# The set-up of a three-stage kernel, reordered: three K buffers, value sums on TensorE, the expert-embedding norm moved into attention, one activation table set, other queue orders

## The reference

```python
# stage A: attention over a window of |i-j| < 16 and 24 block summaries per head
k_sum = k.reshape(B, H, nb, 32, D).max(axis=3)      # 24 blocks of 32 rows
v_sum = v.reshape(B, H, nb, 32, D).mean(axis=3)
scores = concat(masked(q @ k.T / sqrt(D)), q @ k_sum.T / sqrt(D) + log(32))
x = softmax(scores) @ concat(v, v_sum)              # (1536, 512)
# stage B: top-1 of 8 experts
xn, en = x / (norm(x) + 1e-6), expert_emb / (norm(expert_emb) + 1e-6)
expert = argmax(xn @ en.T / tau);  gate = max softmax probability
x = gate * (relu(x @ w1[expert]) @ w2[expert])      # 512 -> 1024 -> 512
# stage C: a rational activation
h = x @ w_in                                        # 512 -> 2048
out = (P(h) / (Q(|h|) + 1e-6)) @ w_out              # -> (1536, 512)
```

## Time and profile before

| | us |
|---|---|
| three runs | 852.5, 858.95, 860.91 |
| median of them | 858.95 |
| profiled execution, whole time | 860.77 |
| its span, first to last instruction | 859.2 |
| PE busy | 711.8 |
| DVE busy | 514.1 |
| ACT busy | 432.4 |
| POOL busy | 162.0 |

### The profile page before, as it was taken

How to read it: one execution, slowest core, us unless ns; L and a number is a source line. 1 busy time by engine, 2 the same in 40 slices (tenths; PEclk the granted TensorE clock), 3 DMA queues, 4 the chain that set the end, 5 groups by cost and what they waited for, 6 DMA issues and landing times.

```text
span 859.2 us, 12541 instructions
## 1 busy us (share of the span) xinstructions
PE 711.8 (83%) x3368; PEld 563.4 (66%) x3369; DVE 514.1 (60%) x922; ACT 432.4 (50%) x783; POOL 162.0 (19%) x210
## 2 busy tenths in 40 slices
PE   0586995999308888889899988479999999999995
PEld 0564774777206666768678767357778677878884
DVE  4861662566503646631331330479999899989996
ACT  3461662466304556532432442466666666666663
POOL 5756662431150000010101000310100000000000
PEclk9785997899658998999989999779999999999999
DMA  6134352440344668730541250210000100010001
GB/s 221 56 114 154 111 143 53 107 104 15 125 180 173 229 229 289 266 127 33 205 161 49 77 187 17 67 56 13 26 13 0 49 0 0 0 50 0 1 2 49
DMA packets 54380, 80.54 MB, mean 94 GB/s; under 512 B 31168, under 2 KB 31168, under 8 KB 53064
## 3 DMA queue, kind: packets, MB, share of 16 engines
q1 hardware_dynamic: 45144, 54.39, 19.7%
q0 software_dynamic: 6112, 20.45, 6.9%
q10 hardware_dynamic: 3088, 5.26, 1.7%
HBM read 63.48 MB, written 16.61 MB: 93 GB/s over the span
## 4 chain that ended last, share of the span: by engine, by line
PE 48%; DVE 19%; DMA 11%; ACT 9%; issue 5%; SPq 3%; POOL 3%; ACTq 1%; DVEq 0%; POOLq 0%
PE bank L1290 13%; PE bank L1117 8%; DMA xg<-x_by_slot 8%; PE bank L1269 6%; PE bank L1343 5%; PE bank L1358 5%; PE bank L1205 3%; SPq L340 3%; PE bank L1179 3%; DVE qd L1073 3%; DVE pb L1075 3%; DVE rr L1074 3%; ACT rr L755 2%; PE bank L1204 2%; DVE qd L1066 2%
## 5 line engine op out<-in xcount | busy, mean ns | idle before, releaser
L1358 PE MATMUL bank<-weights,G 128*128 128x512 f32 x576 | 144.4, 400 | 5.9 <-DVE G L998 5.8
L1343 PE MATMUL bank<-X2T,weights 128*128 (+1 forms) x576 | 145.8, 403 | 1.6 <-DVE X2T L998 1.6
L1358 PEld LDWEIGHTS bank<-weights,G 128*128 128x128 f32 x576 | 108.9, 190 | 34.1 <-DVE G L998 5.7
L1343 PEld LDWEIGHTS bank<-X2T,weights 128*128 128x128 f32 x576 | 109.8, 192 | 28.6 <-issue 2.3
L1290 PE MATMUL bank<-weights,HT 128*128 x456 | 122.2, 428 | 2.4 <-DVE HT L998 2.4
L1269 PE MATMUL bank<-weights,XT 128*128 (+1 forms) x456 | 116.4, 405 | 5.7 <-DVE XT L998 5.7
L1290 PEld LDWEIGHTS bank<-weights,HT 128*128 128x128 f32 x456 | 92.8, 207 | 24.4 <-issue 2.6
L1269 PEld LDWEIGHTS bank<-weights,XT 128*128 128x128 f32 x456 | 85.2, 191 | 27.4 <-issue 8.8
L998 DVE TENSOR_TENSOR HT<-bank,HT 128x512 fp32r<-128x512 f32 x38 | 24.5, 686 | 101.3 <-ACT HT L700 101.2
L755 ACT ACTIVATE rr<-qd,onep 128x512 f32<-128x512 f32 x48 | 34.9, 727 | 51.9 <-DVE qd L1066 51.9
L998 DVE TENSOR_TENSOR weights<-raw_early,weights 128x2048 f32 (+1 forms) x18 | 40.5, 2289 | 32.7 <-ACT weights L679 21.8
(11 more groups left out here) (180 smaller groups left out, 1246.0 us busy)
## 6 DMA issues: line engine op xcount, KB each, us to landing
raw_early<-in_moe_w_dram SPq DMA_DIRECT2D x14, 1024.0 KB, 5.1
raw_late<-in_moe_w_dram SPq DMA_DIRECT2D x14, 1024.0 KB, 8.8
x_by_slot<-x_all ACTq DMA_DIRECT2D x5, 1024.0 KB, 5.1
xg<-x_by_slot POOLq DMA_DIRECT2D x19, 256.0 KB, 5.6
y_by_slot<-yo POOLq DMA_DIRECT2D x19, 256.0 KB, 2.3
x_all<-in_moe_w_dram POOLq DMA_DIRECT2D x8, 512.0 KB, 5.3
kraw<-in_k_dram SPq DMA_DIRECT2D x3, 1024.0 KB, 5.3
qraw<-in_q_dram SPq DMA_DIRECT2D x12, 256.0 KB, 4.6
```

Of the source, the lines that this page charges most:

```text
L1343: last = T_.matmul(bank[6 + f % 2][:, :], W[:, 0, wa, kc * F2 + f * P:kc * F2 + (f + 1) * P], X2T[:, bass.ds(c % 2, 1), xa, kc * C_TOK:(kc ...
L1358: last = T_.matmul(bank[tt][:, :], G[:, f % 2, ga, tt * P:(tt + 1) * P], W[:, 1, wa, f * DM:(f + 1) * DM], start=(f == 0 and n_ == 0), sto ...
```

## The change

Eight edits, all ahead of stage B but one.

1. `kraw` gets three buffers. `load_k(2)` moves up behind `load_q(0)` and waits for nothing. ACT's `key_halves(2)` moves ahead of `key_columns(1)`; DVE's `key_max` is cut in two parts, and `key_max(2)` and `key_maxima(2)` move into the attention loop (DVE units 0 and 1, PE and ACT unit 4).
2. The value sums of groups 0 and 1 move from POOL to PE: four matmuls of 512 columns by the identity into one bank (`value_sums`), and a reduction and a scaling on DVE (`mean_v` on DVE). Group 2 stays on POOL, later.
3. The embedding norm moves into attention: ACT unit 0, DVE units 2 and 3, PE unit 3.
4. `Sqrt` becomes `Ln` and `Exp` with scale 0.5, and one table set is loaded at the start; the load ahead of stage C goes.
5. `DVE_FILLS` goes from two fills of a group to one.
6. POOL: `windows(0)` ahead of `split_q(1)`, `split_q(2)` and `windows(2)` ahead of the constants; the splits of expert 0's weights are spread over tiles 3 to 8, two in tiles 4 and 6.
7. SP: `load_q(T + 1)` ahead of `load_v(T)`.
8. SP: the `VA` load of the first tile of a batch is cut in two, 80 rows and 9.

The scratch row of `square_sum` becomes `x_all[T + 1]`, so `make_x(T)` waits for `ss_done` of T.

```diff
@@ sync
-                if g >= 2:
-                    sp.wait_ge(kmax_ready, g - 1)
-                sp.dma_start(kraw[:, g % 2, :], k_rows[g * P:(g + 1) * P, :]).then_inc(k_in[g], 16)
+                sp.dma_start(kraw[:, g, :], k_rows[g * P:(g + 1) * P, :]).then_inc(k_in[g], 16)
...
+                split = mid if cut == 0 else FIRST_ROWS
+                at = NSUM + split - start
+                sp.dma_start(heads(VA[NSUM + cut:at, r, :]),
+                             v[b, :, start + cut:split, :].rearrange("h p d -> p h d")).then_inc(v_in[r], 16)
+                if split < mid:
+                    sp.dma_start(heads(VA[at:P, r, :]),
+                                 v[b, :, split:mid, :].rearrange("h p d -> p h d")).then_inc(v_in[r], 16)
...
             load_q(0)
+            load_k(2)
             load_v_all(0)
             load_v_all(1)
             load_q(1)
-            load_k(2)
             sp.wait_ge(cleared, 1)
             load_v(0)
             load_v(1)
             store_means(0)
-            load_v_all(2)
             store_means(1)
             load_means(0)
             load_means(1)
+            load_v_all(2)
+            load_q(2)
             store_means(2)
             for T in range(2, NT):
-                load_q(T)
+                if T + 1 < NT:
+                    load_q(T + 1)
                 load_v(T)
@@ gpsimd
             split_q(0)
-            mean_v(0)
-            mean_v(1)
-            split_q(1)
             windows(0, 0)
             windows(0, 1)
+            split_q(1)
             windows(1, 0)
             windows(1, 1)
+            split_q(2)
+            windows(2, 0)
             mean_v(2)
+            windows(2, 1)
             load_raw(0)
             load_raw(1)
...
-            split_slab0(0)
-            for T in range(2, NT):
+            SPLITS = {3: (0,), 4: (1, 2), 5: (3,), 6: (4, 5), 7: (6,), 8: (7,)}
+            for T in range(3, NT):
                 split_q(T)
                 windows(T, 0)
                 windows(T, 1)
-                if T < 2 * CHUNKS + 1:
-                    split_slab0(T - 1)
+                for j in SPLITS.get(T, ()):
+                    split_slab0(j)
@@ scalar
+            A_.preload_act_table_set("natural_log_exp_and_others")
+            def norm_of_embedding():
...
+                A_.activation(sm[0:E, 1:2], sm[0:E, 0:1], ACT.Ln).then_inc(emb_log, 1)
+                act.wait_ge(emb_log, 1)
+                A_.activation(sm[0:E, 1:2], sm[0:E, 1:2], ACT.Exp, scale=0.5).then_inc(emb_root, 1)
...
+            key_halves(2)
             key_columns(1)
             key_maxima(1)
-            key_halves(2)
             key_columns(2)
-            key_maxima(2)
...
+                if u == 0:
+                    norm_of_embedding()
+                if u == 4:
+                    key_maxima(2)
...
-            A_.preload_act_table_set("natural_log_exp_and_others")
@@ vector
+            def mean_v(g):
+                dve.wait_ge(vm_mm, g + 1)
+                link(V.tensor_reduce(vmean[:, g, :], bank[7 - g][:, :].rearrange("p (r d) -> p d r", d=D), AX.X, ALU.add))
+                V.tensor_scalar(vmean[:, g, :], vmean[:, g, :], 1.0 / BLOCK, None, ALU.mult).then_inc(vmean_ready, 1)
+
+            key_lo(0)
+            key_max(0, True, False)
+            key_lo(1)
+            key_column(0, 0)
+            key_max(0, False, True)
+            key_max(1, True, False)
+            mean_v(0)
+            key_lo(2)
+            key_column(1, 0)
+            key_max(1, False, True)
+            mean_v(1)
+            key_column(2, 0)
...
+                if u < 2:
+                    key_max(2, u == 0, u == 1)
+                if u == 2:
+                    scale_embedding()
+                if u == 3:
+                    place_embedding()
@@ tensor
+            def value_sums(g):
+                pe.wait_ge(v_all_in[g], 16)
+                if g == 1:
+                    pe.wait_ge(ks_sb, 1)
+                for j in range(4):
+                    last = T_.matmul(bank[7 - g][:, :], ident[:, :], vraw[g][:, j * BANK:(j + 1) * BANK],
+                                     start=(j == 0), stop=(j == 3))
+                last.then_inc(vm_mm, 1)
...
-            for g in range(KG):
-                key_columns(g)
-                key_maxima(g)
+            key_columns(0)
+            key_maxima(0)
+            value_sums(0)
+            key_columns(1)
+            key_maxima(1)
+            value_sums(1)
+            key_columns(2)
             wait_fills(pe, KG * FILLS)
-            pe.wait_ge(ks_sb, KG)
-            pe.wait_ge(eb_ready, 1)
+            pe.wait_ge(vmean_ready, 2)
+            pe.wait_ge(ks_sb, 2)
...
+                if u == 4:
+                    key_maxima(2)
...
+                if u == 3:
+                    embedding()
```

More of the change, by code:

```diff
@@ L162, in moe_mlp_kernel @@
         zero = x_all[:, NT - 1, :]
-        raw0 = [x_all[:, NT - 6 + 2 * i:NT - 4 + 2 * i, :].rearrange("p t d -> p (t d)") for i in range(2)]
+        vraw = [vraw0[:, :], x_all[:, 0:4, :].rearrange("p t d -> p (t d)")]
+        raw0 = [x_all[:, NT - 5 + 2 * i:NT - 3 + 2 * i, :].rearrange("p t d -> p (t d)") for i in range(2)]
         top_end = Region(raw_at)
@@ L256, in moe_mlp_kernel @@
         FILLS = BLOCK // 4
-        DVE_FILLS = (2, 5)
+        DVE_FILLS = (4,)
+        FIRST_ROWS = 80
         TAIL = 2
@@ L599, in key_maxima @@
                 act.wait_ge(ks_mm, g + 1)
-                A_.copy(KSs[:, g * P:(g + 1) * P], bank[6 + g % 2][:, 0:P]).then_inc(ks_sb, 1)
+                A_.copy(KSs[:, g * P:(g + 1) * P], bank[(6, 7, 7)[g]][:, 0:P]).then_inc(ks_sb, 1)
             key_halves(0)
@@ L643, in square_sum @@
                 act.wait_ge(x_done, T + 1)
-                A_.activation(x_all[:, NT - 2, :] if T < NT - 2 else qraw[:, 0, :], x_all[:, T, :], ACT.Square, accum_out=ss[:, T:T + 1]).then_inc(ss_done, 1)
+                if T + 1 == NT - 5:
+                    act.wait_ge(w0_ready, 2 * CHUNKS)
+                A_.activation(x_all[:, T + 1, :] if T < NT - 2 else qraw[:, 0, :], x_all[:, T, :], ACT.Square, accum_out=ss[:, T:T + 1]).then_inc(ss_done, 1)
             def zero_rows(it):
@@ L670, in _ @@
             act.wait_ge(ss_done, NT)
-            A_.activation(r12[:, 0, 0:NT], ss[:, :], ACT.Sqrt).then_inc(norm_root, 1)
+            A_.activation(r12[:, 0, 0:NT], ss[:, :], ACT.Ln).then_inc(norm_log, 1)
+            act.wait_ge(norm_log, 1)
+            A_.activation(r12[:, 0, 0:NT], r12[:, 0, 0:NT], ACT.Exp, scale=0.5).then_inc(norm_root, 1)
             act.wait_ge(shifted, 1)
@@ L841, in key_column, with key_max @@
                 V.tensor_copy(kt_dst(i), kt_src(i)).then_inc(kt_dve, 1)
-            def key_max(g):
-                t = kraw[:, g % 2, :]
-                w = ROW // 2
+            def key_max(g, first, last):
+                t = kraw[:, g, :]
                 dve.wait_ge(k_lo, 2 * g + 2)
-                link(V.tensor_tensor(t[:, 0:w], t[:, 0:w], t[:, w:2 * w], ALU.max))
-                key_column(g * FILLS + DVE_FILLS[0])
-                while w > 2 * D:
-                    w //= 2
+                if first:
+                    w = ROW // 2
@@ L1119, in _, with embedding @@
             pe.wait_ge(ident_ready, 1)
-            pe.wait_ge(en_ready, 1)
-            for kc in range(KC):
-                last = transpose(bank[7][:, kc * E:(kc + 1) * E], en[:, kc * P:(kc + 1) * P], E)
-            last.then_inc(eT_mm, 1)
+            def embedding():
+                pe.wait_ge(en_ready, 1)
+                wait_qs(pe, 4)
+                for kc in range(KC):
+                    last = transpose(bank[6][:, kc * E:(kc + 1) * E], en[:, kc * P:(kc + 1) * P], E)
+                last.then_inc(eT_mm, 1)
+            def value_sums(g):
[6 more added lines that the diff above has]
+                last.then_inc(vm_mm, 1)
             def key_columns(g):
@@ L1139, in key_maxima @@
                 if g == 1:
-                    pe.wait_ge(eb_ready, 1)
-                if g >= 2:
-                    pe.wait_ge(ks_sb, g - 1)
-                transpose(bank[6 + g % 2][:, 0:P], KMX[:, g, :, :].rearrange("p a d -> p (a d)").bitcast(F32))\
+                    pe.wait_ge(vmean_ready, 1)
+                if g == 2:
+                    wait_qs(pe, 5)
+                transpose(bank[(6, 7, 7)[g]][:, 0:P], KMX[:, g, :, :].rearrange("p a d -> p (a d)").bitcast(F32))\
                     .then_inc(ks_mm, 1)
-            for g in range(KG):
-                key_columns(g)
-                key_maxima(g)
+            key_columns(0)
[5 more added lines that the diff above has]
+            key_columns(2)
             wait_fills(pe, KG * FILLS)
-            pe.wait_ge(ks_sb, KG)
-            pe.wait_ge(eb_ready, 1)
+            pe.wait_ge(vmean_ready, 2)
+            pe.wait_ge(ks_sb, 2)
             def query_stack(u):
@@ L1160, in query_stack @@
                     pe.wait_ge(x_done, (u - 10) // 4 + 1)
+                if u == 6:
```

(3 more changed lines are left out.)

83 lines of the change are left out of this document (44 added, 39 removed).

## The result

| | before | after |
|---|---|---|
| median (lowest to highest), us | 856.53 (852.5 to 860.91) | 830.22 (827.92 to 832.66) |
| executions | 4 | 4 |
| span of the profiled execution | 859.2 | 826.4 |
| mean granted clock | 0.915 | 0.936 |
| DVE, ACT, POOL, PE busy | 514.1, 432.4, 162.0, 711.8 | 511.7, 427.4, 143.8, 707.8 |

The account below looks back on a forecast made before the run. PE was taken as bound, held up by set-up and two waits for POOL's queries behind a blocked SP queue. Terms of -10.2, +4.1, +4.5, -31.5, +1 and -2.3 on 859.2 gave 824.8, stated as 826, range 815 to 842.

Parts of the forecast that it names:

- Stalls: Attention, 62.70 to 158.13 us: PE's two waits for POOL's query splits go and 22 units run at full pace, -31.5 us.
- The cut load doesn't help: Rival for SP's VA load: 80 rows still run on one engine, SP held some 12 us twice; +4, 830; chance 0.05.
- Set-up: Before attention: earlier K work and fills bring the first scores at 40.3 instead of 50.51, -10.2 us (-11.5 to -6.5).
- Units 0 to 4: First attention units: work moved onto DVE makes scores(4) come 11.2 us after scores(0), not 7.08; +4.1 (+2.4 to +6.6).
- The clock: First attention units: PE works some 1.7 us of 5, so one fall to 0.50 is expected; +4.5 us (0 to +7.5).
- The clock doesn't fall: Rival for the first attention units: DVE's chain is at its short end and the clock holds; 820; chance 0.15.
- PE stays at 1.2 GHz: Rival, slower than before: after the sparse first units DVE paces PE at the low clock; 928 at ten tiles; chance 0.02.
- POOL: Attention: query splits finish 0.7 to 3 us before PE wants them; +1 us (0 to +10) for one that slips.
- Tables: ACT: two table loads of 1.28 us on the path go and one short activation is added; -2.3 us.
- Stage B and C: After attention: these stages fall differently against the clock and the expert loads, of either sign; chance 0.08.
- the four amounts named: Low end of the range: 1.3, 1.7, 4.5 and 2 off 826, from low bounds of set-up and clock; about 815.
- no SP issue over 2 us: Sign expected in the changed profile: no SP transfer issue takes over 2 us, and no DMA share of 0.08 for long.

Follow-up runs that it names:

- the kernel with filler: Six extra identity matmuls of 512 columns, results unused, in PE's unit 3 of the changed kernel; 822.07 us against 852.24 before, one execution.
- the two padded kernels: Changed kernel with 16 or 32 one-column DVE memsets ahead of its first wait; 822.77 us against 854.98, and 822.39 against 852.24, one execution each.

## Why the prediction was right

The forecast was 826 in a range of 815 to 842; the median is 830.22, and the profiled span 826.4 against a forecast of 824.8 for it. By the terms of the sum:

- **Stalls: forecast -31.5, measured -31.6.** Both are gone for the reason named. SP isn't held by the 80 rows and 9 rows, and the experiment with the cut alone shows that this by itself brings all but 1.2 us. "The cut load doesn't help" is refuted by issues of 0.32 to 0.44 us. The Trainium skill ("DMA: Bandwidth & Descriptors", Why a DMA increments its semaphore by 16 and not by 1) had the divisor rule, one engine for 89 rows and sixteen for 80; the share of 0.08 in the earlier trace rows and the short issues after the cut agree with it.
- **Set-up: forecast -10.2, measured -12.0, outside its bounds of -11.5 to -6.5.** The walk held at its steps: fills from 8.65 (8.8), maxima of group 0 at 17.46 (16.9), value sums ending at 23.0 (24.2) and 32.9. What was priced too high were the value sums: 5.21 with the clock low for half of it and 3.61 at full clock, where I had 6.8 for the first. At full clock it is 3.64, in the kernel with filler. That is near the lower bound of 3.4. The third group's fills took 3.66, where I had 5.2 to 6.5. In the four executions with a full clock at `value_sums(0)` and the norm in attention, the first scores came at 36.7 to 37.0, so the term is -13.5 to -13.8 in them.
- **Units 0 to 4: forecast +4.1, measured +7.4, outside its bounds of +2.4 to +6.6.** This is the term that was mis-sized. The failed step is the price of DVE's small instructions: I took six short steps of 1.2 in all and allowed only for the 8 x 512 scaling and the step behind it to be slow beside POOL. In the trace after, the work that moved into attention takes DVE 9.8 us, where I had 5.9 to 8.6. Of that, `key_max(2)` is 5.0 (3.4 in the forecast), its second part beside POOL's split of the queries, and the six short steps are 2.6, beside POOL's adds of V, which run from 46.69 to 52.17. One operation on 8 numbers took 1.69 instead of 0.15, the constant of two columns 0.68, and the subtraction of the maxima 1.22 instead of 0.22. I had walked DVE's queue without laying POOL's queue beside it. The kernel before showed the effect: its 5.46 us of the same adds were in the earlier trace rows, and the same small step (its L813) took 0.77 there beside POOL's split of the queries. The other executions of the same DVE work show that POOL is the cause, because another instruction is long each time. With 16 stores ahead, `key_max(2)` was done before POOL began, and its subtraction took 0.22. The small step took 1.21 and ended at 45.33, as POOL's split did (45.32), and the two-column constant took 2.29 and ended at 48.68, as POOL's first add did (48.66). The term was +6.4 and +6.3 in the two padded kernels, at the upper end of the bounds: by how much it lies outside depends on what meets what.
- **The clock: forecast +4.5, measured +4.2.** The fall came at about 48 us and lasted to about 62. The kernel with filler turns it off and gets the 4.2 back. The closeness of the number is partly luck: the padded kernels, with the same PE program, lost 1.6 and 1.5. "The clock doesn't fall" was thus a possible outcome of a small step, and "PE stays at 1.2 GHz" was refuted: 63 us at 1.00 follow. The Trainium skill ("TensorE: Matmul & The Clock Gate", Part 1: The HAM clock gate) has the idle state as the throttled one. The trace agrees by the lengths of the matmuls: PE's first transposes took 421 ns from 8.6 to 11.9 and 272 later, and in the kernel before 421 ns from 20.3 to 22.9. I had read the 1.00 of the earlier trace rows against the rule, and that reading was wrong. It cost the forecast little. The first eight fills took 6.32 against 3.66 for the third group's, but the 5.21 of the earlier trace rows that I took for them had the slow start in it already, and ACT was free to copy them only from 11.73 on. What the column does show is the fall at 17 to 18 us, behind a wait of 2.50.
- **POOL: forecast +1, measured 0.** From 62 to 186 us PE waits for nobody. The margins of 0.7 to 3 us were enough in tiles 4 and 6 too, which hold two weight splits.
- **Tables: forecast -2.3, measured -1.0 for the first.** The last logits to the scatter is 1.0 shorter: one load of 1.28 less and one activation of 0.21 more. (Another load went with it, at 223.58 in the kernel before; ACT waited 1.49 us for DVE behind that one, so it cost nothing.) The second load can't be told: it lies in stage B, whose length varied between 307.1 and 317.0 over the kernels without it (mean of eight 310.2) and between 310.6 and 314.5 over the kernels with it (mean of four 312.4). No drain beside a load was seen, at 1.28 each.
- **Stage B and C: given 0.08 for a difference of either sign, and no term in the sum.** Stage B gave some 3.9 and stage C took 4.1, so the sum came out right with two terms missing that cancel. The first is within what stage B varies by. The second isn't noise: it is the stop at DVE's jump back, and the shift by 16 instructions takes it away. I had named a change of over 3 us in B or C as what would make the prediction wrong; by that measure it was, in two places, with opposite signs. That they cancel is luck. The 826.4 of the profiled execution hits the 824.8 more closely than the terms do: set-up gained 1.8 more, units 0 to 4 lost 3.3 more, POOL didn't lose its 1.0, and the tables gained 1.3 less.

Put together: the set-up edits gained 12.0 and gave back 11.6 by u = 6, and SP's edits gained 31.6. The forecast had this in kind (-10.2, +4.1, +4.5 against -31.5), and the experiments make it firm for SP's edits: those two alone have 0.9741, everything has 0.9692. The lower end of the range was added up wrongly: 826 less the four amounts named is 816.5, not 815.

One thing on the list of what would show it was too strict: "no SP issue over 2 us". In set-up after, SP's issue of `VA` at 7.84 took 7.42 us, with the DMA share at 0.85 and 305 GB/s: there the engines were full. PE never waited for a transfer there. A long issue means trouble only with a low DMA share beside it.

## What to carry to other kernels

Where a queue is blocked by an issue of many microseconds while the DMA share is a sixteenth, look at the row count of the transfer ahead of it: a cut into two that divide was worth 26.8 us at u = 28 here, more than the whole reordering around it. Work that is moved out of a set-up isn't hidden for being somewhere else: if the loop that receives it is paced by the same engine, it comes back there (12.0 gained, 7.4 and then 4.2 of clock given back); lay it in pieces of about a microsecond over several rounds (14.7 us instead of 23.7 for six units here), and lay the timeline of the other engines beside each small instruction. After any edit that changes the number of instructions of an engine, look at its first instruction behind each loop's jump back.

## What the runs showed of the hardware

- DVE's jump back in stage C costs either no more than a step within the loop (0.61 us from start to start) or 4.90 us beyond it, for the same loop body, and 16 more instructions far ahead of it decide which. In the trace it has no releaser, only two register instructions with 2.93 and 2.44 us behind them.
- A small DVE instruction beside an add or a subtraction of two tensors on POOL can last until POOL's instruction ends, whatever its own size. On 8 x 1 numbers it took 1.69 us and ended at 49.05, where POOL's add on 128 x 1024 ended at 49.03; with 16 stores ahead a constant of 128 x 2 took 2.29 and ended at 48.68, POOL's add at 48.66. In the changed kernel the next one of the same kind took 0.15 although POOL's row of five adds ran on to 52.17.
- The clock column reads 1.00 ahead of PE's first work and in it, yet the first transposes took 421 ns each, as at 0.50 (418), against 272 later, in the kernel before as in the changed one. The length of a single matmul is the better witness there.
- The clock of the same stretch of the same PE and DVE work fell to 0.50 in some executions and not in others: `value_sums(0)` took 5.21 in the changed kernel and 3.64 in the one with filler, which is the same program up to there, behind waits of 2.50 and 3.30 us. The fall in the first units cost 4.2 us in the changed kernel and 1.6 and 1.5 in the two padded ones. The clock term of a forecast is worth a range, even where PE's program is the same.
